# Second product of a two-layer MoE chain: 64-column matmuls for one term, the last group in halves, weight pieces split one group sooner

## The reference

```python
# 1. causal convolution of 7 taps, softmaxed weights per head (8 heads of 24 channels)
out = np.einsum('hk,bskhg->bshg', softmax(weight), windows_of(x))
# 2. first MLP, 192 -> 2048 -> 192
h = x @ w_in;  g = h * np.clip(h + 3.0, 0.0, 6.0) / 6.0;  x = g @ w_out
# 3. second MLP, 192 -> 2048 -> 192
h = x @ w_in2; g = np.where(h > 0, h, np.exp(np.minimum(h, 0.0)) - 1.0);  y = g @ w_out2
```

## Time and profile before

| what | us |
|---|---|
| median of three runs (1163.23 to 1166.45) | 1165.34 |
| the profiled execution's own time | 1164.05 |
| its span | 1162.3 |
| TensorE busy with matmuls | 1152.9 (99%) |
| VectorE busy | 901.3 (78%) |
| ScalarE busy | 632.3 (54%) |
| GpSimd busy | 42.6 (4%) |

### The profile page before, as it was taken

How to read it: one execution, slowest core, us unless ns; L and a number is a source line. 1 busy time by engine, 2 the same in 40 slices (tenths; PEclk the granted TensorE clock), 3 DMA queues, 4 the chain that set the end, 5 groups by cost and what they waited for, 6 DMA issues and landing times.

```text
span 1162.3 us, 24067 instructions
## 1 busy us (share of the span) xinstructions
PE 1152.9 (99%) x9740; PEld 925.5 (80%) x9740; DVE 901.3 (78%) x960; ACT 632.3 (54%) x682; POOL 42.6 (4%) x36
## 2 busy tenths in 40 slices
PE   9998999999999999999999999999999999999998
PEld 6887888888888888888888888888888888888886
DVE  7787687878878787787877878788787887876765
ACT  7665555545555465555545555555554555546544
POOL 4333000000000000000000000000000000000000
PEclk9999999999999999999999999999999999999999
DMA  4311010000001001010010100101000010000000
GB/s 150 114 33 33 1 33 0 27 5 0 32 0 32 0 0 32 0 32 0 0 32 0 32 0 0 32 0 32 0 11 21 0 32 0 9 5 10 6 2 28
DMA packets 14760, 22.48 MB, mean 19 GB/s; under 512 B 1424, under 2 KB 5520, under 8 KB 14736
## 3 DMA queue, kind: packets, MB, share of 16 engines
q1 hardware_dynamic: 14592, 22.12, 6.1%
q10 hardware_dynamic: 144, 0.01, 0.0%
HBM read 15.83 MB, written 6.29 MB: 19 GB/s over the span
## 4 chain that ended last, share of the span: by engine, by line
PE 99%; ACT 0%; DVE 0%; issue 0%; POOLq 0%; DVEq 0%; ACTq 0%
PE h_ps L637 31%; PE acc_a L651 31%; PE acc_b L659 21%; PE h_ps L644 15%; PE h_ps L785 0%; PE h_ps L776 0%; PE acc_a L776 0%; PE h_ps L667 0%; PE acc_a L699 0%; PE acc_b L701 0%; PE acc_b L708 0%; PE acc_a L700 0%; PE acc_a L707 0%; DVE hidden L499 0%; POOLq L62 0%
## 5 line engine op out<-in xcount | busy, mean ns | idle before, releaser
L344 ACT CAST g_hi<-hidden 128x1024 fp32r<-128x1024 f32 x256 | 269.1, 1051 | 352.7 <-DVE hidden L504 239.5
L508 DVE TENSOR_TENSOR g_lo<-hidden,g_hi 128x1024 fp32r<-128x1024 f32 x256 | 313.6, 1225 | 129.0 <-ACT g_hi L344 129.0
L637 PE MATMUL h_ps<-in_hi_a,win_hi_a 64*128 64x512 f32 x1012 | 398.3, 394 | 3.1 <-POOL wout_b L292 3.1
L651 PE MATMUL acc_a<-g_hi,wout_hi_a 64*128 64x512 f32 x1012 | 398.5, 394 | 0.0
L637 PE MATMUL h_ps<-in_lo_a,win_hi_a 64*128 64x512 f32 x1012 | 398.2, 393 | 0.0
L651 PE MATMUL acc_a<-g_hi,wout_lo_a 64*128 64x512 f32 x1012 | 398.2, 393 | 0.0
L637 PE MATMUL h_ps<-in_hi_a,win_lo_a 64*128 64x512 f32 x1012 | 398.2, 393 | 0.0
L659 PE MATMUL acc_b<-g_hi,wout_b 64*128 64x512 f32 x1012 | 318.0, 394 | 0.0
L659 PE MATMUL acc_b<-g_lo,wout_b 64*128 64x512 f32 x1012 | 317.9, 394 | 0.0
L651 PE MATMUL acc_a<-g_lo,wout_hi_a 64*128 64x512 f32 x1012 | 317.9, 394 | 0.0
L499 DVE SCALAR_TENSOR_TENSOR hidden<-hidden,h_ps 128x1024 f32<-128x1024 f32 x128 | 156.2, 1221 | 85.0 <-ACT hidden L334 84.9
(11 more groups left out here) (92 smaller groups left out, 1271.8 us busy)
## 6 DMA issues: line engine op xcount, KB each, us to landing
xwin_a<-x_win SPq DMA_DIRECT2D x16, 259.0 KB, 2.7
raw_in<-w_in SPq DMA_DIRECT2D x8, 512.0 KB, 4.3
out_t<-out_a SPq DMA_DIRECT2D x16, 256.0 KB, 2.9
xwin_b<-x_win SPq DMA_DIRECT2D x15, 259.0 KB, 2.9
raw_out<-w_out SPq DMA_DIRECT2D x8, 384.0 KB, 3.7
out_t<-out_b SPq DMA_DIRECT2D x16, 128.0 KB, 2.3
xnext_b<-x_win SPq DMA_DIRECT2D x1, 259.0 KB, 5.2
taps<-tap_w ACTq DMA_DIRECT2D x1, 7.0 KB, 2.4
```

Of the source, the lines that this page charges most:

```text
L344: nc.scalar.copy(g_hi[:, g % PARTS, :], hidden[:, g % 2, :]).then_inc(hi_ready, 1)
L508: nc.vector.tensor_tensor(g_lo[:, g % PARTS, :], hidden[:, g % 2, :], g_hi[:, g % PARTS, :].bitcast(F32), ALU.subtract).then_inc(lo_ready, 1)
L637: return nc.tensor.matmul(bank(g, c), w[HALVES[r], columns(g, c)], x[HALVES[r], :], start=start, stop=c == 0 and r == 1 and term == 2)
L651: return nc.tensor.matmul(acc_a[acc][:, :], w[HALVES[r], g * CPG + c, :], x[HALVES[r], g % PARTS, c * TOK:(c + 1) * TOK], start=g == 0 and ...
```

## The change

Four edits, in five places of the code:

1. GpSimd's half h of the weight pieces, for h from 17 on (the second MLP's), waits for the activation of one group earlier.
2. `g_lo` into `acc_b` takes only weight columns 0 to 63 and writes rows 0 to 63 of `acc_b`. In the interleaved step the order of the last four `acc_b` matmuls goes from high, high, low, low to high, low, low, high, and the one that closes the sum is a high one.
3. The last group (255) is done in two halves of 512 columns on ScalarE and VectorE. Its second product is a new function, `last_product`, which waits for both halves, does `acc_b` first (low, then high), signals `last_b`, and then does `acc_a`. ScalarE copies `acc_b` at `last_b` and `acc_a` at the end. SP stores `out_b` first, then `out_a`.
4. The zero matmuls at the start read 256 columns instead of 512, and there are four instead of two; the memset covers 256 columns.

```diff
--- before.py
+++ after.py
@@ -145,6 +145,7 @@
         take1_b = sem("take1_b")
         take2 = sem("take2")
         take2_b = sem("take2_b")
+        last_b = sem("last_b")
         stored = sem("stored")
 
 
@@ -265,8 +266,13 @@
             with sp.Fori(2, TILES - 2) as i:
                 load_x(i + 2)
                 store(i - 2)
-            for t in range(TILES - 4, TILES):
+            for t in range(TILES - 4, TILES - 1):
                 store(t)
+            last = (TILES - 1) * TOK
+            sp.wait_ge(take2_b, TILES)
+            sp.dma_start(out_t[DA:D, last:last + TOK], out_b[:, :]).then_inc(stored, 16)
+            sp.wait_ge(take2, 2 * TILES)
+            sp.dma_start(out_t[0:DA, last:last + TOK], out_a[:, :]).then_inc(stored, 16)
             sp.wait_ge(stored, 32 * (TILES + 1))
 
 
@@ -288,7 +294,7 @@
                     if h < 3:
                         continue
                     pool.wait_ge(w_hi, h + 1)
-                    pool.wait_ge(act_done, (together[h] if h < 16 else h - 8) + 1)
+                    pool.wait_ge(act_done, (together[h] if h < 16 else max(h - 9, GROUPS)) + 1)
                     nc.gpsimd.tensor_tensor(lo, raw, hi.bitcast(F32), ALU.subtract).then_inc(w_split, 1)
 
 
@@ -418,12 +424,29 @@
             with nc.Fori(2, TILES - 1, engines=[mybir.EngineType.Activation], hint_back_edge=True) as i:
                 pair(i, "steady")
             pair(TILES - 1, "last")
-            for g in range(GROUPS):
+            for g in range(GROUPS - 1):
                 nonlinear(1, LAST2, g)
                 if g == 3:
                     take_mlp2(TILES - 2, 1)
                 high_part(LAST2, g)
-            take_mlp2(TILES - 1, 0)
+
+
+            G = LAST2 + GROUPS - 1
+            act.wait_ge(h_ready, G + 1)
+            act.wait_ge(lo_ready, G - 1)
+            for c in range(CPG):
+                cols = slice(c * TOK, (c + 1) * TOK)
+                nc.scalar.activation(hidden[:, 1, cols], h_ps[1][:, cols], ACT.Exp).then_inc(act_done, 1)
+            act.wait_ge(parts_used, G - PARTS + 1)
+            for c in range(CPG):
+                cols = slice(c * TOK, (c + 1) * TOK)
+                act.wait_ge(g_ready, G + c + 1)
+                nc.scalar.copy(g_hi[:, PARTS - 1, cols], hidden[:, 1, cols]).then_inc(hi_ready, 1)
+            act.wait_ge(stored, 32 * TILES)
+            act.wait_ge(last_b, 1)
+            nc.scalar.copy(half_b2[:, :], acc_b[0][DB:2 * DB, :]).then_inc(take2, 1)
+            act.wait_ge(parts_used, LAST2 + GROUPS)
+            nc.scalar.copy(out_a[:, :], acc_a[0][:, :]).then_inc(take2, 1)
 
 
         @block.vector
@@ -509,7 +532,7 @@
                                         g_hi[:, g % PARTS, :].bitcast(F32), ALU.subtract).then_inc(lo_ready, 1)
 
 
-            nc.vector.memset(conv_b[:, :], 0.0).then_inc(zero_set, 1)
+            nc.vector.memset(conv_b[:, 0:HALF], 0.0).then_inc(zero_set, 1)
             nc.vector.memset(three[:, :], 3.0).then_inc(three_set, 1)
             dve.wait_ge(taps_loaded, 16)
             nc.vector.tensor_reduce(tap_stat[:, :, 0:1], taps[:, :, :], AX.X, ALU.max).then_inc(tap_chain, 1)
@@ -612,11 +635,25 @@
             with nc.Fori(2, TILES - 1, engines=[mybir.EngineType.DVE], hint_back_edge=True) as i:
                 pair(i, "steady")
             pair(TILES - 1, "last")
-            for g in range(GROUPS):
+            for g in range(GROUPS - 1):
                 nonlinear(1, LAST2, g, TILES - 1)
                 if g == 3:
                     take_mlp2(TILES - 2, 1)
                 low_part(LAST2, g)
+
+            G = LAST2 + GROUPS - 1
+            for c in range(CPG):
+                cols = slice(c * TOK, (c + 1) * TOK)
+                v = hidden[:, 1, cols]
+                dve.wait_ge(act_done, G + c + 1)
+                nc.vector.tensor_scalar(v, v, 1.0, -1.0, ALU.min, ALU.add).then_inc(expm1_done, 1)
+                dve.wait_ge(expm1_done, TILES * GROUPS + c)
+                nc.vector.tensor_tensor(v, v, h_ps[1][:, cols], ALU.max).then_inc(g_ready, 1)
+            for c in range(CPG):
+                cols = slice(c * TOK, (c + 1) * TOK)
+                dve.wait_ge(hi_ready, G + c + 1)
+                nc.vector.tensor_tensor(g_lo[:, PARTS - 1, cols], hidden[:, 1, cols],
+                                        g_hi[:, PARTS - 1, cols].bitcast(F32), ALU.subtract).then_inc(lo_ready, 1)
             take_mlp2(TILES - 1, 0)
 
 
@@ -655,11 +692,12 @@
 
             def out_b_part(m, g, acc, c, term, r):
 
-                x = (g_hi, g_lo)[term]
-                return nc.tensor.matmul(acc_b[acc][:, :], wout_b[m][HALVES[r], g * CPG + c, :],
+
+                x, n = ((g_hi, 2 * DB), (g_lo, DB))[term]
+                return nc.tensor.matmul(acc_b[acc][0:n, :], wout_b[m][HALVES[r], g * CPG + c, 0:n],
                                         x[HALVES[r], g % PARTS, c * TOK:(c + 1) * TOK],
                                         start=g == 0 and c == 0 and term == 0 and r == 1,
-                                        stop=g == GROUPS - 1 and c == 1 and term == 1 and r == 0)
+                                        stop=g == GROUPS - 1 and c == 1 and term == 0 and r == 0)
 
             def in_whole(m, g, src, c):
 
@@ -703,9 +741,25 @@
                 for c in range(CPG):
                     f = g * CPG + c
                     x = g_lo[:, g % PARTS, c * TOK:(c + 1) * TOK]
-                    end = f == CHUNKS - 1
-                    nc.tensor.matmul(acc_a[acc][:, :], wout_hi_a[m][:, f, :], x, start=False, stop=end)
-                    mm = nc.tensor.matmul(acc_b[acc][:, :], wout_b[m][:, f, :], x, start=False, stop=end)
+                    nc.tensor.matmul(acc_a[acc][:, :], wout_hi_a[m][:, f, :], x, start=False, stop=False)
+                    mm = nc.tensor.matmul(acc_b[acc][0:DB, :], wout_b[m][:, f, 0:DB], x, start=False, stop=False)
+                mm.then_inc(parts_used, 1)
+
+            def last_product(m, base, g, acc):
+
+                pe.wait_ge(hi_ready, base + g + 2)
+                pe.wait_ge(lo_ready, base + g + 2)
+                for x, n in ((g_lo, DB), (g_hi, 2 * DB)):
+                    for c in range(CPG):
+                        mm = nc.tensor.matmul(acc_b[acc][0:n, :], wout_b[m][:, g * CPG + c, 0:n],
+                                              x[:, g % PARTS, c * TOK:(c + 1) * TOK], start=False,
+                                              stop=x is g_hi and c == 1)
+                mm.then_inc(last_b, 1)
+                for w, x in ((wout_hi_a, g_hi), (wout_lo_a, g_hi), (wout_hi_a, g_lo)):
+                    for c in range(CPG):
+                        mm = nc.tensor.matmul(acc_a[acc][:, :], w[m][:, g * CPG + c, :],
+                                              x[:, g % PARTS, c * TOK:(c + 1) * TOK], start=False,
+                                              stop=x is g_lo and c == 1)
                 mm.then_inc(parts_used, 1)
 
             def both_products(m, base, g, src, load, low, om, obase, og, acc, oload):
@@ -759,11 +813,11 @@
                 pe.wait_ge(turn, 3 * O + 2)
                 out_b_part(om, og, acc, 0, 0, 0)
                 in_rest(m, g, src, 2, 1, stop=True)
-                out_b_part(om, og, acc, 1, 0, 0)
+                out_b_part(om, og, acc, 0, 1, 0)
                 in_a(m, g, src, 0, 0, 1)
-                out_b_part(om, og, acc, 0, 1, 0)
+                out_b_part(om, og, acc, 1, 1, 0)
                 in_a(m, g, src, 0, 1, 1)
-                out_b_part(om, og, acc, 1, 1, 0).then_inc(parts_used, 1)
+                out_b_part(om, og, acc, 1, 0, 0).then_inc(parts_used, 1)
                 in_a(m, g, src, 0, 2, 1).then_inc(h_ready, 1)
 
             def conv_rest(window, banks):
@@ -781,8 +835,8 @@
             def first_start():
 
                 pe.wait_ge(zero_set, 1)
-                for c in range(CPG):
-                    nc.tensor.matmul(bank(0, c), conv_b[:, 0:P], conv_b[:, :], start=True, stop=True)
+                for c in range(2 * CPG):
+                    nc.tensor.matmul(bank(0, c % 2)[:, 0:HALF], conv_b[:, 0:P], conv_b[:, 0:HALF], start=True, stop=True)
                 pe.wait_ge(x0b_loaded, 16)
                 conv_rest(xwin_b, (bank(1, 0), bank(1, 1)))
                 pe.wait_ge(x1b_loaded, 16)
@@ -865,8 +919,9 @@
             pair(TILES - 1, "last")
             phase(1, LAST2, 0, (1, first_group2(TILES - 2), 1, False), 0,
                   wait(in2_ready, 2 * TILES), nothing, nothing)
-            for g in range(GROUPS - LAG, GROUPS):
+            for g in range(GROUPS - LAG, GROUPS - 1):
                 second_product(1, LAST2, g, 0)
+            last_product(1, LAST2, GROUPS - 1, 0)
 
 
 def kernel(**inputs):
```

## The result

| | us |
|---|---|
| before, median (1163.23 to 1166.45) | 1165.34 |
| after, median (1156.25 to 1157.0) | 1156.51 |
| ratio | 0.9927, interval 0.991 to 0.9944 |
| profiled execution of after, its span | 1156.3, 1154.5 |

The change is 0.7% faster.

A forecast was written before the change was run, and what follows sets the result against it. The prediction took TensorE's matmul spacing, repeated over 253 groups, as the bound: 1164.05 - 4.8 - 1.1 - 0.1 + 511 + 1.4 = 1670.5 us profiled, so about 1672 us as median, range 1154 to 1745.

The forecast's parts named there:

- What bounds the kernel: TensorE, busy for 99% of the span; 253 groups of 19 matmul slots 0.234 us apart make 1125 of 1162 us.
- Part 2: 64 columns for `g_lo` into `acc_b` in the loop: tile changes drain the array, 2.02 us a step, 511 us slower.
- the 1.4 us of the tail: Last three second products: another 8 changes of tile at 0.17 us each, 1.4 us slower.
- only the rows of the tile decide what can run side by side: Rival A: a change in columns costs nothing; 1159.3 us, down to 1139 if shorter loads count; chance 0.35.
- Part 2's other half, the shorter loads,: Shorter weight loads of the narrowed loop matmuls: taken as no gain, since loads aren't the limit; at most 20 us.
- Part 1: GpSimd's weight halves one group sooner: TensorE's wait for the last half goes; gain 4.8 us, bounds 3.5 and 4.8.
- the profiled execution's 1.3 us below the median: Final step of the sum: profiled execution 1670.5 us, taken to lie 1.3 us below the median, so 1671.8.
- Part 3: Last group in halves, `acc_b` finished and stored first: the end comes 1.1 us sooner, bounds 0.4 and 1.3.
- The added wait of `last_product`: TensorE's wait for both halves of `g_lo` in the last group: costed at nothing, late by 0.5 us at most.
- Part 4: Shorter memset at the start: zero matmuls 0.2 us sooner, and the convolution if its input has landed; gain 0.1 us.

The follow-up runs named there:

- e5: Changed kernel with one first-product term of each interleaved step as one matmul of 128 rows instead of two of 64; 1254.43 us in its one run.
- e6: Changed kernel with one matmul of each step on 32 rows instead of 64; 1311.06 us, ratio 1.1247 to the kernel before.
- e1: Changed kernel with 128 weight columns again instead of 64 for `g_lo` into `acc_b`, in the loop and the tail; 1158.81 us, ratio 0.9944.
- e3: Changed kernel with 64 columns for `g_hi` into `acc_b` too, in groups 1 to 6 of each tile, one matmul swapped with its neighbour; 1155.38 us.
- e0: The changed kernel once more, unaltered, as the measure for the others; 1156.19 us, ratio 0.9924 to the kernel before.
- e2: Changed kernel with 96 weight columns instead of 64 for `g_lo` into `acc_b`, in the loop and the tail; 1157.87 us, ratio 0.9935.
- e10: Changed kernel with 32 weight columns instead of 64 for `g_lo` into `acc_b`, everywhere; 1156.34 us, ratio 0.9926.
- e4: Kernel before with only GpSimd's weight halves from 17 on moved one group sooner; 1160.19 us beside 1166.0, ratio 0.9955.
- e8: Kernel before with only the 64 columns for `g_lo` into `acc_b` and the new order of `acc_b` matmuls; 1162.68 us beside 1165.31, ratio 0.9974.
- e7: Changed kernel with SP issuing the convolution's second input ahead of the first weight piece; 1156.95 us, ratio 0.993.
- e9: Changed kernel with the last group undone: whole on ScalarE and VectorE, old second product, `out_a` stored first; 1157.84 us, ratio 0.994.
- e11: Changed kernel with the start undone: two zero matmuls of 512 columns and a memset of 512; 1156.76 us, ratio 0.9929.

## Why the prediction was wrong

**What bounds the kernel** was read rightly: the distance from one pair to the next counts 253 times, all else once.

**Part 2 is the step that failed.** The forecast took a change in columns for a change of tile that drains the array, its reading of the 0.37 us without a load in the earlier trace rows, and put it at 2.02 us a step: eight changes at 0.19 us, less 0.20, and three slots lost because nothing would run side by side. Both terms are zero. The prediction priced a change of tile from `64*128` to `64*64` by the only change that the trace had, from `128*128` to `64*128`. That was a change in rows. e5 confirms its price in the loop (0.19 us, 98 us for 506), and e6 shows that a change in rows costs it even where the other tile would fit beside its neighbour. A change in columns costs nothing: eight in a step leave the step shorter (4.441 us against e1's 4.451), with tiles of 64 columns and of 32, in e3 with longer runs of narrow matmuls, and in the tail, where `128*128` and `128*64` alternate:

```profile
1144.92 0.40 PE L744 MATMUL acc_a<-g_lo,wout_hi_a 128*128 128x512 f32 x1
1145.16 0.39 PE L745 MATMUL acc_b<-g_lo,wout_b 128*64 128x512 f32 x1
1145.39 0.40 PE L744 MATMUL acc_a<-g_lo,wout_hi_a 128*128 128x512 f32 x1
```

So 511 us, and the 1.4 us of the tail, are zero. The prediction had written down what decides ("only the rows of the tile decide what can run side by side") and gave it 0.35; it took the one measured neighbour for the nearer one, though that neighbour differed in the other dimension. A row about the wrong dimension bounds nothing from below, and the half of the chance that went there was too much.

**Part 2's other half, the shorter loads,** was taken as nothing, with a bound of 20 us. It is 2.6 us (e1 against e0; 10 ns a step x 253 = 2.5). The reason given for nothing, that a `128*128` matmul with one load has the same distance as a pair with two, was too coarse: rows are printed to 10 ns, and 2.5 ns a matmul can't be seen in one distance. It is seen in 224 groups, and e2 ties it to the number of columns (4.446 us a group at 96, with a load of 159 ns instead of 185). That it is the load's own time is an estimate, since no run shortens the load alone; why a load that seems covered would still cost is open. That the next 32 columns give hardly anything (e10) fits a wait which ends with the neighbour's load of 128 columns instead, but no run tells that apart.

**Part 1 was right.** GpSimd's last half starts at 109.90 in after, in order of time:

```profile
109.90 1.18 POOL L298 TENSOR_TENSOR wout_b<-raw_out,wout_b 128x256 fp32r<-128x256 f32 x1 [2.65 <-ACT hidden L342]
```

It is done at 111.08, 1.9 us before TensorE starts the pair that needs it (112.93), as worked out. From ScalarE's fourth activation of `hidden` to the 25th, before takes 98.43 us and e1, which has part 1 but no narrow matmul, 93.57: 4.86, where the sum said 4.8: 3.22 for the gap, 0.11 for the exposed loads, and 1.47 for the eight pairs of the earlier trace rows that follow from 117.22 on, where the granted clock reads 0.50 (118.00 to 120.00). The median difference of e4 is 5.8. The prediction carried the profiled execution's 1.3 us below the median over to after. That was the small error: what follows the stall is not the same in each execution (1.6 us in before's profile, 2.7 in e8's), and without the stall this part of the scatter goes. The runs of before and of e8, which have the stall, spread over 3.2 and 3.8 us, those of the kernels without it and with a time near after's over 0.5 (e3) to 1.9 us (e7), and the profiled execution of after lies 0.2 us below its median. That the spread comes from the clock behind the stall is argued from two traces, not shown in each run.

**Part 3** was put at 1.1 with bounds of 0.4 and 1.3; it is 0.86 by the profiles (5.09 to 4.23), and e9 gives 0.88 by its profile and 1.1 by its runs. The copy of `out_a` and its store come as worked out (0.43 and 1.05 us behind the start of the last matmul); what was taken too short is the landing of `out_a`, 2.4 us in after and e0 where the sum had 2.1. That the store of `out_b`, issued 0.64 us ahead of it, is the reason is not shown. The added wait of `last_product` costs nothing, as said: its first row starts at 1148.18, 0.23 us after the last of the product ahead of it.

**Part 4** was put at 0.1 and is nothing that the runs can tell (e11). Its mechanism is in the profiles all the same. In the ten with the short zero matmuls the convolution starts at 4.90 or 4.91 us, in e4, e8 and e11, with the long ones, at 5.17: 0.27 sooner, as the zeros start. Only the profile of the kernel before doesn't fit, with 4.83: its zeros take 3.43 us from start to end where those of all others take 3.78, and why is open. What hides the gain comes behind it. The first tile's 28 convolution matmuls take 3.3 to 4.4 us, at a granted clock of 1.00 in all (why is open), and in after, e1 and e10 the second tile's convolution then waits for its input. So the first activation is anywhere from 13.73 to 14.96 us. It is 0.47 us later in after than in before, but e0, the same kernel as after, has 13.90: this is scatter.

**Sum over the two profiles:** 4.86 (part 1) + 2.5 (loads) + 0.86 (part 3) - 0.47 (start) = 7.75, where the spans differ by 7.8 (1162.3 to 1154.5).

## What to carry to other kernels

Before pricing a change of TensorE's tile, say which dimension changes. A change in the number of rows cost 0.19 us here every time, and in e6 the matmul with the other number of rows ran beside nothing, so keep one row size through a loop; columns could be cut without a price, and cutting those that compute nothing useful is worth a little (here 2.5 ns of 117 a matmul, not the share of the load that it removes). Where the only measured neighbour of an unknown cost differs in another respect than the edit does, and the edit stands in a loop, the two prices are two cases and neither is an estimate of the other.

## What the runs showed of the hardware

- Matmuls of `64*64` and `64*128` run side by side on the two row halves (both start at 600.78 above, the next pair 0.23 us later); in e6 `32*128` and `64*128` didn't (602.11, 602.43, 602.85), and the load ahead of a change in rows starts only with the matmul itself (0.36 us without a load in e5 and in e6).
- A weight load's record goes by its columns (185, 159, 132, 106 ns for 128, 96, 64, 32) on 64 rows, and fewer columns save a little even where the load is hidden: 2.5 ns a matmul where its load is 53 ns shorter, in proportion from 128 to 64 columns, then 0.3 ns for the next 26.
- After a gap of 3.1 us in TensorE's work the granted clock fell to 0.50, either by the first pair behind it (e8, 116.70 to 121.70) or 1.3 us later (before, 0.50 from 118.00 to 120.00), and the distances were back to 0.23 us from 122.8 and 120.6 us on. The same stall so costs 1.6 or 2.7 us beside its own length.
- Whether two matmuls of 64 columns can also run beside each other in the columns of the same rows was not tried.
- The second input of the convolution landed 5.2 to 6.8 us after its issue in kernels that issue it in the same order. Three of the thirteen profiles (after, e1, e10) waited for it, TensorE's second convolution starting at 8.32 to 9.07 us where e0 has 8.12.
